# Bucketed attention before two feed-forward layers: q and k brought feature first, one-hot rows replaced by sign-bit rows, scores copied to SBUF by VectorE

## The chip, the cores and the metric

The kernel runs on one core of one Trainium2 chip. The metric is the device time of one execution in microseconds. The kernel before takes 830.13 us (median of three runs, 829.33 to 830.82).

## What is computed

For each of 2 x 8 heads of 768 rows and 64 features, a six-bit bucket is formed of every q row and every k row (the signs of six projections). Row i may attend to column j only if the buckets are equal. The result goes through two feed-forward layers of 1536 tokens, 512 to 2048 to 512.

```python
q_bits = (einsum('bhsd,dk->bhsk', q, proj) > 0)       # k_bits likewise
mask = q_bucket[:, :, :, None] == k_bucket[:, :, None, :]
scores = where(mask, scale * q @ k.T, -1e9)
attn = exp(scores - max(scores)); attn /= (attn.sum(-1) + 1e-9)
x = (attn @ v) heads side by side                     # (1536, 512)
h = x @ w_in;  g = where(h > 0, h, exp(min(h, 0)) - 1);  x = g @ w_out
h = x @ w_in2; g = s * relu(h) ** 2 + b;                 out = g @ w_out2
```

## The kernel before

Every fp32 product is made of fp32r parts: a value is split into `hi` (rounded to fp32r) and `lo` (the rest), and two or three products of parts are summed. Five engine programs are written by hand and meet at counting semaphores; the order on each engine is the order of the text.

**Units and pairs.** The attention part runs over 8 pairs of heads (`PAIRS`). A pair is 12 units (`UNITS`), six blocks of 128 query rows for each of its two heads; `k` is the unit in the pair, `u` the unit in all. In unit `k` TensorE does: the scores of unit `u + 2` (`AHEAD`), four matmuls of 384 columns (`scores`, L449); the transposes of the probabilities of unit `u`, six fp32 blocks of 128x128 in two groups of three (`transpose_probs`, L461); and then, by `third = k % 3`, either the turn of a finished value product (`turn`, L485; `third` 0) or half of the value product of the three units before (`times_v`, L470; six matmuls of 384 columns; `third` 1 and 2). A unit with the turn is called a turn unit here, the others value units.

**Buffers in PSUM.** `s_ps` has two buffers of two banks, `pt_ps` two of one bank, `pv_ps` and `prep_ps` one bank each: eight in all. Scores of `u` wait for the exponential of `u - 2` (L452).

**Per unit on the other engines.** VectorE takes the minimum of each row of the (negated) scores out of PSUM (`row_minimum`, L752), ScalarE reads the scores from PSUM again and writes the exponentials to `probs` (`exp`, L647, with the row sum as accumulator output). The transposed halves leave PSUM in two steps each: ScalarE copies `pt_hi` (L627), VectorE subtracts `pt_lo` (L759), so two pairs of evictions of 384 columns a unit.

**Preparation of the next head.** A table `PLAN` spreads eight cycles over three places of each unit: q and k are transposed through `prep_ps` (QA, QB, KA, KB: three fp32r transposes each, L429), projected (ZA, ZB: eight matmuls, L434), their signs stored as `bits` (L744), and two small bf16 products (EA, EB, L439) count the equal bits for every bucket; ScalarE makes one-hot rows of q (L640) and VectorE mismatch rows of k times 2^60 (L747), so that the score product itself adds 2^60 where the buckets differ. Three DMAs inside SBUF copy rows (`copy_hi`, L273). GpSimd (POOL) splits q, k and v and one block of feed-forward weights a pair. The x transposes (L446) bring a pair's result into `xt_hi` (ScalarE) and `xt_lo` (VectorE, L793), in units 3 and 9.

**End of a group.** After each three units VectorE inverts the row sums (`invert`, L765 and L767) and, behind the turn, multiplies them in (`normalise`, L776).

```python
        elif cycle <= ZB:
            for j, x in enumerate((qt1, qt1, kt2, kt2)):
                last = mm(dst, planes[:, n, j, :], x[par][:, cols], ...)
...
    ts(kt2[par][DH:P, cols], bank[0:BUCKETS, 0:HALF], equal_at, BIG, ALU.not_equal, ALU.mult)
...
    ts(row_inv[:, c], row_sum[:, c], EPS, None, ALU.add)
```

**The feed-forward layers** take 2304 matmuls of 512 columns (`hidden` L492, `output` L507). Four hidden blocks (12 matmuls each) of the first chunk are worked in at the end of the attention part, in units of the drain after the last pair (`FILL`, and one more behind the last x transposes). ScalarE and VectorE turn each hidden block into `g_hi` and `g_lo` (Relu, Exp, g, L877, L879), for which `output` waits.

Of the kernel before, what the change touches and what calls it, by code (L numbers as in the profile page):

```python
# [64 lines left out]

C_ID, C_II, C_CODE, C_THR, C_END = 0, P, P + DH, 2 * P + DH, 2 * P + DH + 1


def constants():

    c = np.zeros((P, C_END), np.float32)
    c[:, C_ID:C_ID + P] = np.eye(P)  # L90
    c[:, C_II:C_II + DH] = np.tile(np.eye(DH), (2, 1))
    bit = (np.arange(BUCKETS)[None, :] >> np.arange(BITS)[:, None]) & 1
    for start in (0, BIT_ROWS):
        c[start + BITS:start + 2 * BITS, C_CODE:C_CODE + BUCKETS] = 4 * bit - 2
        c[start:start + BITS, C_CODE + BUCKETS:C_CODE + 2 * BUCKETS] = 4 * bit - 2
    equal = BITS + (2 * bit - 1).sum(0)
    c[0:BUCKETS, C_THR] = equal
    c[BUCKETS:, C_THR] = 1 - equal
    return c

# [8 lines left out]
def build(nc, q, k, v, proj, consts, w1_in, w1_out, w2_in, w2_out, s2, b2, out):  # L109
    ctx = ExitStack()  # L110
    with ctx:
# [11 lines left out]
        ident_r = sb("ident_r", [P, P], F32R)  # L123
        code = sb("code", [P, P], BF16)
# [8 lines left out]
        equal_at = cst[0:BUCKETS, C_THR:C_THR + 1]  # L133
        onehot_bias = cst[BUCKETS:P, C_THR:C_THR + 1]
# [779 lines left out]
```

## Time and profile before

| | |
|---|---|
| median of 3 runs | 830.13 us (829.33 to 830.82) |
| span of the profiled execution, first to last instruction | 824.9 us |
| PE / DVE / ACT / POOL busy | 809.9 / 445.3 / 364.7 / 181.0 us |
| granted TensorE clock, mean | 1.000 of full speed |
| attention part | from the start to about 290 us |
| feed-forward layers | from about 290 us to the end |

The profile shows one execution. Its only time of its own is the span; what lies around it is not in the page, and the runs' median is 5.2 us above it. Busy shares are averages over two parts with different needs: in the attention part VectorE and ScalarE are busy for most of the time, in the layers for a third and a quarter of it.

### The profile page before, as it was taken

The page shows a single profiled execution, that of the slowest core. Times are in us where ns is not written, and L with a number is a line of the kernel's source. Part 1 is how long each engine was busy: PE and PEld are TensorE (multiplying, and loading weights), DVE is VectorE, ACT ScalarE, POOL GpSimd, SP SyncE. Part 2 cuts the span into 40 slices and gives each one's busy share as a digit, 9 for nine tenths or more (in the row PEclk, how much of TensorE's full clock was granted, in tenths as well). Part 3 has the DMA queues.
Part 4 walks back from the last instruction along what each step waited for, and adds up shares of the span by engine and source line. Part 5 has one row for each costly group of instructions (what it writes and reads, how often), then busy time and mean ns, then how long its engine had stood idle before and what let it go on. Part 6 is the DMA issues. An engine that isn't in the chain of part 4 may idle for free.

```text
span 824.9 us, 12868 instructions
## 1 busy us (share of the span) xinstructions
PE 809.9 (98%) x4252; PEld 697.6 (85%) x4252; DVE 445.3 (54%) x780; ACT 364.7 (44%) x735; POOL 181.0 (22%) x160
## 2 busy tenths in 40 slices
PE   7999999999999999999999999999999999999998
PEld 6799999999999977888888888887888888888886
DVE  6888888888888839533333343335223432243323
ACT  4888888888888831123221222213221222222221
POOL 3243332334322209400000036663000000000000
PEclk9999999999999999999999999999999999999999
DMA  3423243232323013200000012330000100010001
GB/s 97 120 59 94 76 103 91 57 92 74 87 68 88 1 52 125 80 1 0 1 1 1 0 33 94 102 102 26 1 1 0 51 0 0 0 51 0 0 0 51
DMA packets 34359, 38.70 MB, mean 47 GB/s; under 512 B 3168, under 2 KB 25824, under 8 KB 34336
## 3 DMA queue, kind: packets, MB, share of 16 engines
q1 hardware_dynamic: 33744, 38.22, 16.0%
q8 instruction: 15, 0.25, 0.1%
q10 hardware_dynamic: 592, 0.17, 0.1%
q14 instruction: 8, 0.07, 0.0%
HBM read 26.38 MB, written 3.15 MB: 36 GB/s over the span
## 4 chain that ended last, share of the span: by engine, by line
PE 94%; DVE 3%; DMA 1%; ACT 1%; issue 0%; SPq 0%; ACTq 0%; DVEq 0%
PE acc L521 31%; PE h_ps L503 31%; PE pt_ps L466 8%; PE s_ps L457 4%; PE pv_ps L479 4%; PE pv_ps L480 4%; PE s_ps L458 4%; PE prep_ps L434 2%; PE pv_ps L489 2%; PE prep_ps L429 2%; PE prep_ps L439 1%; DVE g_lo L879 1%; PE prep_ps L446 1%; DVE pt_lo L759 1%; DMA qt<-qt 0%
## 5 line engine op out<-in xcount | busy, mean ns | idle before, releaser
L721 ACT ACTIVATE r_sb<-h_ps 128x512 f32<-128x512 f32 x96 | 57.4, 598 | 359.4 <-PE h_ps L503 359.4
L873 DVE TENSOR_SCALAR g_sb<-e_sb,sb_scale 128x512 f32<-128x512 f32 x48 | 26.2, 546 | 158.1 <-ACT e_sb L724 158.1
L759 DVE TENSOR_TENSOR pt_lo<-pt_ps,pt_hi 128x384 fp32r<-128x384 f32 x192 | 103.4, 552 | 13.2 <-ACT pt_hi L627 11.3
L871 DVE SCALAR_TENSOR_TENSOR g_sb<-e_sb,h_ps 128x512 f32<-128x512 f32 x48 | 32.9, 686 | 132.2 <-ACT e_sb L724 132.2
L627 ACT ACTIVATE pt_hi<-pt_ps 128x384 fp32r<-128x384 f32 x192 | 93.4, 494 | 24.5 <-PE pt_ps L466 23.7
L752 DVE TENSOR_REDUCE row_min<-s_ps 128x1 f32<-128x768 f32 x96 | 91.4, 953 | 21.0 <-PE s_ps L458 20.5
L466 PE MATMUL pt_ps<-cst,probs 128*128 128x128 f32 x576 | 95.8, 277 | 1.5 <-DVE pt_lo L759 1.5
L647 ACT ACTIVATE probs<-s_ps,row_min 128x768 f32<-128x768 f32 x96 | 86.7, 904 | 0.9
L879 DVE TENSOR_TENSOR g_lo<-g_sb,g_hi 128x512 fp32r<-128x512 f32 x96 | 80.5, 838 | 3.3
L466 PEld LDWEIGHTS pt_ps<-cst,probs 128*128 128x128 f32 x576 | 68.6, 140 | 12.4 <-issue 6.0
L503 PE MATMUL h_ps<-xt_hi,wa_hi 128*128 (+1 forms) x192 | 75.1, 391 | 0.4 <-DVEq L856 0.4
L503 PE MATMUL h_ps<-xt_hi,wa_lo 128*128 (+1 forms) x192 | 74.8, 389 | 0.0
L503 PE MATMUL h_ps<-xt_lo,wa_hi 128*128 (+1 forms) x192 | 74.7, 389 | 0.0
L503 PE MATMUL h_ps<-xt_hi,wb_hi 128*128 (+1 forms) x192 | 74.7, 389 | 0.0
L503 PE MATMUL h_ps<-xt_lo,wb_hi 128*128 (+1 forms) x192 | 74.7, 389 | 0.0
L503 PE MATMUL h_ps<-xt_hi,wb_lo 128*128 (+1 forms) x192 | 74.7, 389 | 0.0
L479 PE MATMUL pv_ps<-pt_hi,v_nat 128*128 128x384 f32 x192 | 70.4, 366 | 0.6 <-DVE w_raw L776 0.6
L457 PE MATMUL s_ps<-kt,qt 128*128 128x384 f32 x192 | 68.4, 356 | 2.5 <-ACT qt L640 1.3
L724 ACT ACTIVATE e_sb<-r_sb 128x512 f32<-128x512 f32 x96 | 60.7, 632 | 11.0 <-ACT r_sb L721 0.8
L480 PE MATMUL pv_ps<-pt_lo,v_nat 128*128 128x384 f32 x192 | 64.8, 338 | 0.0
L458 PE MATMUL s_ps<-kt,qt 128*128 128x384 f32 x192 | 64.5, 336 | 0.0
L361 POOL CAST wa_hi<-w_raw 128x1024 f32 (+1 forms) x16 | 17.6, 1103 | 157.1 <-PE acc L521 157.1
(118 smaller groups left out, 1613.2 us busy)
## 6 DMA issues: line engine op xcount, KB each, us to landing
w_raw<-w_in_dram SPq DMA_DIRECT2D x32, 256.0 KB, 2.8
w_raw<-w_out_dram SPq DMA_DIRECT2D x32, 256.0 KB, 2.9
kt<-kt SPq DMA_DIRECT2D x30, 192.0 KB, 2.9
raw_q<-q_dram SPq DMA_DIRECT2D x16, 192.0 KB, 2.4
raw_k<-k_dram SPq DMA_DIRECT2D x16, 192.0 KB, 2.5
raw_v<-v_dram SPq DMA_DIRECT2D x16, 192.0 KB, 2.4
out_dram<-o_sb SPq DMA_DIRECT2D x12, 256.0 KB, 2.1
qt<-qt SPq DMA_DIRECT2D x15, 192.0 KB, 3.7
```

What stands on the lines that cost most here:

```text
L457: mm(s_ps[buf][:, n, 0:HALF], q1, kt1[par][:, cols], start=True, stop=False)
L458: last = mm(s_ps[buf][:, n, 0:HALF], q2, kt2[par][:, cols], start=False, stop=True)
L466: last = nc.tensor.transpose(pt_ps[n][:, r * P:(r + 1) * P], probs[k % 2][:, (n * HT + r) * P:(n * HT + r + 1) * P], ident)
L479: mm(pv_ps[:, 0:HALF], v_nat[par][:, kt, :], pt_hi[buf][:, kt, :], start=kt == 0, stop=False)
L480: last = mm(pv_ps[:, 0:HALF], v_nat[par][:, kt, :], pt_lo[buf][:, kt, :], start=False, stop=kt == TILES - 1)
L503: last = mm(bank[:], w[a][:, kt * P:(kt + 1) * P], x[b], start=n == 0, stop=n == 3 * KT - 1)
L521: last = mm(acc[n][:], lhs, rhs, start=f == 0 and j == 0, stop=f == FT - 1 and j == 2)
L627: return nc.scalar.activation(dst, src, ACT.Copy, scale=scale)
L647: nc.scalar.activation(probs[k % 2][:].rearrange("p (n c) -> p n c", n=2), s_ps[k % 2][:, :, 0:HALF], ACT.Exp, bias=row_min[:, k:k + 1], s ...
L752: nc.vector.tensor_reduce(row_min[:, k:k + 1], s_ps[k % 2][:, :, 0:HALF], AX.XY, ALU.min).then_inc(min_done, 1)
L759: tt(pt_lo[(k // HT) % 2][where], pt_ps[n][:, 0:HALF].rearrange("p (t c) -> p t c", t=HT), pt_hi[(k // HT) % 2][where].bitcast(F32), ALU.s ...
L879: tt(lo[:], g[:], hi[:].bitcast(F32), ALU.subtract).then_inc(g_ready, 1)
```

## The change

- **Host.** q and k arrive transposed and one under the other (`qk`, 64 rows of k, 64 rows of q, 768 columns), v and the planes of the projection laid out. One load a head instead of two.
- **TensorE** loses the q and k transposes, two of the eight projection matmuls a head (`project`: planes_hi and planes_lo by kt1, planes_hi by kt2) and the one-hot products. `project` stands at the end of units 1 and 7, the x transposes at the end of units 4 and 5.
- **Masking.** Instead of one-hot rows, twelve rows of sign bits times 2^31 lie in `qt2` and `kt2`; their product adds 2^62 for every bit that differs. VectorE writes them in four instructions of 12x384 (`write_bits`, units 2, 3, 8 and 9).
- **Scores.** `s_ps` has one buffer of two banks. VectorE copies the scores to `probs` (three buffers) under a ceiling of 2^60 and gives the row minimum as accumulator output of the same instruction (`keep_scores`); ScalarE takes the exponential in place, from SBUF. Scores of `u` wait for `keep_scores` of `u - 1`.
- **Evictions.** `pt_ps` has two buffers of two banks; a unit has one copy `pt_hi` and one subtraction `pt_lo` of 768 columns.
- **Moves.** `normalise` goes from VectorE (one instruction) to ScalarE (three of 64 columns); x is kept by ScalarE as fp32 (`keep_x`) and split by GpSimd (`split_x`); GpSimd scales q, splits q and k together. The inverse's first step becomes a scalar_tensor_tensor with a second tensor of zeros.
- **SP** copies q's high part twice, q's low part and k's high part once a head.
- **Ends.** Head 0 is split by ScalarE and VectorE in place; the last pair takes hidden blocks 0 and 1 in the place of scores, and blocks 2 and 3 around the last turns; none stands behind the last x transposes.

```diff
-        s_ps = [pb(f"s_ps{n}", [P, 2, 512], att_ps) for n in range(2)]
-        pt_ps = [pb(f"pt_ps{n}", [P, 512], att_ps) for n in range(2)]
+        s_ps = pb("s_ps", [P, 2, 512], att_ps)
+        pt_ps = [pb(f"pt_ps{n}", [P, 1024], att_ps) for n in range(2)]
...
 # GpSimd
+                nc.gpsimd.tensor_scalar(raw[low, :], raw[low, :], -SCALE, 1.0, ALU.mult, ALU.mult).then_inc(q_scaled, 1)
+                wait(pool, scores_done, TILES * (head - 1))
+                nc.gpsimd.tensor_copy(kt1[par][:], raw[:]).then_inc(qk_hi, 1)
+                nc.gpsimd.tensor_tensor(kt2[par][:], raw[:], kt1[par][:].bitcast(F32), ALU.subtract).then_inc(qk_split, 1)
...
 # TensorE
-                wait(pe, exp_done, u - 1)
+                wait(pe, scores_kept, u)
...
+                    if (k + AHEAD) % TILES == 0:
+                        pe.wait_ge(q_copied, 48 * head)
+                        pe.wait_ge(k_copied, 16 * head)
+                        pe.wait_ge(bits_done, 4 * head + 3)
+                    if (k + AHEAD) % TILES == HT:
+                        pe.wait_ge(bits_done, 4 * head + 4)
...
 # ScalarE
+                if third == 1 and not (first and k < 2 * HT):
+                    normalise(i, k // HT - 2)
+                if k < UNITS - 1 or more:
+                    exp(u + 1, (k + 1) % UNITS)
+                if third == 0 and not (first and k < 2 * HT):
+                    keep_pv(i, k // HT - 2)
+                split_hi(u, k)
+                if k in X_UNIT and not first:
+                    keep_x(i - 1, X_UNIT[k])
...
 # VectorE
+                ts(dst[DH:DH + 2 * BITS, n * HALF:(n + 1) * HALF], prep_ps[rows, 0:HALF], cst[rows, C_THR:C_THR + 1],
+                   BIT_SIZE, ALU.is_gt, ALU.mult).then_inc(bits_done, 1)
...
+                ts(probs[k % SRING][:].rearrange("p (n c) -> p n c", n=2), s_ps[:, :, 0:HALF], CEILING, HUGE, ALU.min,
+                   ALU.min, accum_out=row_min[:, k:k + 1]).then_inc(scores_kept, 1)
...
-                ts(row_inv[:, c], row_sum[:, c], EPS, None, ALU.add).then_inc(inv_step, 1)
+                nc.vector.scalar_tensor_tensor(row_inv[:, c], row_sum[:, c], EPS, zeros, ALU.add, ALU.add).then_inc(sum_done, 1)
...
+                    keep_scores(u + AHEAD, (k + AHEAD) % UNITS)
+                if blocks:
+                    write_bits(2 * i + off, off % 2, blocks[0])
+                split_lo(u, k)
+                if blocks:
+                    write_bits(2 * i + off, off % 2, blocks[1])
+                if third == 2:
+                    invert(i, k // HT)
```

How the order moves, first on VectorE. Before, units 1 and 2 of a pair (here the last), from the row minimum of unit 1 to the inverse of unit 2:

```order
L752 TENSOR_REDUCE row_min<-s_ps 128x1
L759 TENSOR_TENSOR pt_lo<-pt_ps,pt_hi 128x3x128
L747 TENSOR_SCALAR kt_1<-prep_ps,cst 64x384
L759 TENSOR_TENSOR pt_lo<-pt_ps,pt_hi 128x3x128
L752 TENSOR_REDUCE row_min<-s_ps 128x1
L759 TENSOR_TENSOR pt_lo<-pt_ps,pt_hi 128x3x128
L747 TENSOR_SCALAR kt_1<-prep_ps,cst 64x384
L759 TENSOR_TENSOR pt_lo<-pt_ps,pt_hi 128x3x128
L765 TENSOR_SCALAR row_inv<-row_sum 128x3
L767 RECIPROCAL row_inv<-row_inv 128x3
```

After, units 2 and 3 of the last pair, all that VectorE does in them:

```order
L721 TENSOR_SCALAR probs,row_min<-s_ps 128x768
L714 TENSOR_SCALAR kt_1<-prep_ps,cst 12x384
L728 TENSOR_TENSOR pt_lo<-pt_ps,pt_hi 128x6x128
L714 TENSOR_SCALAR kt_1<-prep_ps,cst 12x384
L734 SCALAR_TENSOR_TENSOR row_inv<-row_sum,cst 128x3
L736 RECIPROCAL row_inv<-row_inv 128x3
L721 TENSOR_SCALAR probs,row_min<-s_ps 128x768
L714 TENSOR_SCALAR qt_1<-prep_ps,cst 12x384
L728 TENSOR_TENSOR pt_lo<-pt_ps,pt_hi 128x6x128
L714 TENSOR_SCALAR qt_1<-prep_ps,cst 12x384
```

The four instructions that make a head's mask rows now stand in two neighbouring units instead of three, and the third of them, for which TensorE waits in unit 4, stands behind two copies of scores, a subtraction and the inverse.

Then TensorE: unit 0 of the last pair before, with the projection of the next head between transposes and turn,

```order
L466 MATMUL pt_ps<-cst,probs 128x128 x3
L434 MATMUL prep_ps<-qt_1,planes 128x384 x2
L434 MATMUL prep_ps<-kt_1,planes 128x384 x2
L466 MATMUL pt_ps<-cst,probs 128x128 x3
L489 MATMUL pv_ps<-cst,pv_sb 128x64 x3
L434 MATMUL prep_ps<-qt_1,planes 128x384 x2
L434 MATMUL prep_ps<-kt_1,planes 128x384 x2
```

and after, the end of unit 1, where the projection now stands (the rows before it are the transposes and the value matmuls of that unit):

```order
L448 MATMUL pt_ps<-cst,probs 128x128 x6
L461 MATMUL pv_ps<-pt_hi,v_nat 128x384
...
L416 MATMUL prep_ps<-kt_1,planes_hi 128x384
L417 MATMUL prep_ps<-kt_1,planes_lo 128x384
L416 MATMUL prep_ps<-kt_1,planes_hi 128x384
L417 MATMUL prep_ps<-kt_1,planes_lo 128x384
L422 MATMUL prep_ps<-kt_1,planes_hi 128x384 x2
```

The projection moved from unit 0 to the end of unit 1 and reads kt_1 alone, in which k and q now lie together.

## Rows read from the trace of the kernel before

**Rows 1.** The page: the span
```profile
span 824.9 us, 12868 instructions
```

**Rows 2.** Windows, 150 to 190 us: us busy (instructions), clock, DMA
```profile
core 0: us, PE busy (x) PEld busy (x) DVE busy (x) ACT busy (x) POOL busy (x), PEclk, DMA share, GB/s
150.00:190.00 40.00, 40.00 (x283) 37.54 (x282) 33.75 (x64) 33.65 (x77) 16.88 (x18) 1.00 0.32 87
```

**Rows 3.** Timeline, PE: start us, length us, engine, line, operation, out<-in, count
```profile
141.08 0.34 PE L457 MATMUL s_ps<-kt,qt 128*128 128x384 f32 x1
146.74 0.34 PE L457 MATMUL s_ps<-kt,qt 128*128 128x384 f32 x1
147.76 0.49 PE L446 MATMUL prep_ps<-cst,w_raw 128*128 128x128 f32 x3
148.09 0.49 PE L466 MATMUL pt_ps<-cst,probs 128*128 128x128 f32 x3
149.00 0.42 PE L457 MATMUL s_ps<-kt,qt 128*128 128x384 f32 x1
176.11 0.34 PE L457 MATMUL s_ps<-kt,qt 128*128 128x384 f32 x1
...
280.83 0.34 PE L457 MATMUL s_ps<-kt,qt 128*128 128x384 f32 x1
281.01 0.34 PE L458 MATMUL s_ps<-kt,qt 128*128 128x384 f32 x1
283.25 0.34 PE L457 MATMUL s_ps<-kt,qt 128*128 128x384 f32 x1
```

**Rows 4.** Timeline, DVE at 146 to 148 us, PE and DVE at 162 us
```profile
146.26 0.61 DVE L747 TENSOR_SCALAR kt<-prep_ps,cst 64x384 fp32r<-64x384 f32 x1
146.90 0.56 DVE L759 TENSOR_TENSOR pt_lo<-pt_ps,pt_hi 128x384 fp32r<-128x384 f32 x1
147.38 0.18 DVE L765 TENSOR_SCALAR row_inv<-row_sum 128x3 f32<-128x3 f32 x1
147.69 0.96 DVE L752 TENSOR_REDUCE row_min<-s_ps 128x1 f32<-128x768 f32 x1
...
161.82 0.34 PE L458 MATMUL s_ps<-kt,qt 128*128 128x384 f32 x1
162.19 0.96 DVE L752 TENSOR_REDUCE row_min<-s_ps 128x1 f32<-128x768 f32 x1 [0.16 <-PE s_ps L458]
```

**Rows 5.** Timeline, POOL, 147 to 149 us
```profile
147.04 0.50 POOL L352 CAST v_nat<-raw_v 128x384 fp32r<-128x384 f32 x1 [13.21 <-PE pv_ps L480]
147.62 1.00 POOL L354 TENSOR_TENSOR v_nat<-raw_v,v_nat 128x384 fp32r<-128x384 f32 x1
148.57 0.50 POOL L335 CAST q_nat<-raw_q 128x384 fp32r<-128x384 f32 x1
```

**Rows 6.** Timeline, POOL and DVE, then tile g_lo (ns, min/median/max)
```profile
312.76 2.40 POOL L363 TENSOR_TENSOR wb_lo<-w_raw,wb_hi 128x1024 f32 x1 [0.17 <-POOL wb_hi L361]
312.91 2.80 DVE L879 TENSOR_TENSOR g_lo<-g_sb,g_hi 128x512 fp32r<-128x512 f32 x1
L879 DVE TENSOR_TENSOR g_lo<-g_sb,g_hi x96: 691/693/2803, 306.8 to 816.0; 128x512 fp32r<-128x512 f32 x96
```

**Rows 7.** Groups of instructions: total busy us, mean ns of one, idle before
```profile
L647 ACT ACTIVATION_READ_ACCUMULATOR probs<-s_ps,row_min 128x1 f32 x96 | 19.5, 203 | 0.0
```

**Rows 8.** Timeline of the start: first cast of q, first and third unit's score matmuls
```profile
4.37 0.36 DVE L820 CAST q_nat<-raw_q 128x384 fp32r<-128x384 f32 x1 [0.21 <-DMA raw_k<-k_dram]
12.67 0.41 PE L457 MATMUL s_ps<-kt,qt 128*128 128x384 f32 x1 [1.27 <-ACT qt L640]
16.50 0.44 PE L457 MATMUL s_ps<-kt,qt 128*128 128x384 f32 x1 [1.21 <-ACT probs L647]
```

**Rows 9.** Timeline, PE: the first output matmul of the feed-forward layers
```profile
307.53 0.50 PE L521 MATMUL acc<-g_hi,wa_hi 128*128 128x512 f32 x1 [0.95 <-DVE g_lo L879]
```

**Rows 10.** The page's DMA issues: count, KB each, us to landing
```profile
kt<-kt SPq DMA_DIRECT2D x30, 192.0 KB, 2.9
```

More of the change, by code:

```diff
@@ L91, in constants, with laid_planes @@
     c[:, C_II:C_II + DH] = np.tile(np.eye(DH), (2, 1))
[L92 to L98, printed above, removed]
-    return c
+    for start in range(0, P, 2 * BIT_ROWS):
+        c[start + BITS:start + 2 * BITS, C_THR] = -TINY
+        c[start + BIT_ROWS:start + BIT_ROWS + BITS, C_THR] = -TINY
+    return c
+def laid_planes(proj):
+    c = np.zeros((P, 2, 2, P), np.float32)
+    for n in range(2):
+        q, k = n * 2 * BIT_ROWS, n * 2 * BIT_ROWS + BIT_ROWS
+        for first, sign in ((0, -1), (BITS, 1)):
+            for rows, at in ((slice(DH, P), q + first), (slice(0, DH), k + first)):
+                c[rows, 0, n, at:at + BITS] = proj
+                c[rows, 1, n, at:at + BITS] = sign
+    return c.reshape(P, 4 * P)
 def wait(eng, sem, value):
@@ L300, in _ @@
                 pair(i)
[L301 to L304 removed]
+            pair(PAIRS - 2, after=False)
+            pair(PAIRS - 1, nxt=False, after=False)
             sp.wait_ge(xt_pe, 2 * PAIRS)
@@ L577, in _ @@
+                if k in Z_UNIT and (more or Z_UNIT[k] < 2):
+                    if k > TILES and not first:
+                        pe.wait_ge(x_kept, 2 * i)
+                    project(2 * i + Z_UNIT[k], Z_UNIT[k] % 2)
             pe.wait_ge(zeros_ready, 1)
@@ new lines, in keep_pv, with normalise @@
+            def keep_pv(i, g):
+                act.wait_ge(pv_done, GROUPS * i + g + 1)
+                copy(pv_sb[:], pv_ps[:, 0:HALF]).then_inc(pv_copied, 1)
+            def normalise(i, g):
+                par, G, first = (g % GROUPS) // 2, GROUPS * i + g, (g % GROUPS) * HT
+                act.wait_ge(inv_done, G + 1)
+                act.wait_ge(pv_turned, G + 1)
+                if g in (0, 1):
+                    wait(act, xt_pe, 2 * i - 1 + g)
+                for r in range(HT):
+                    last = copy(x_nat[:, (g % 2) * HT + r, par * DH:(par + 1) * DH], pv_ps[:, r * DH:(r + 1) * DH],
+                                row_inv[:, first + r:first + r + 1])
+                last.then_inc(x_done, 1)
@@ new lines, in _ @@
+            nc.scalar.activation(row_sum[:, 0:1], qk_scale[:], ACT.Exp)
+            act.wait_ge(k0_in, 16)
+            act.wait_ge(q0_in, 16)
+            for n in range(2):
+                cols = slice(n * HALF, (n + 1) * HALF)
+                copy(kt1[0][:, cols], raw[:, cols], qk_scale[:]).then_inc(hi0_done, 1)
+            act.wait_ge(hi0_done, 2)
+            copy(qt1[0][top, :], kt1[0][low, :].bitcast(F32)).then_inc(q0_copied, 1)
+            copy(qt2[0][top, :], kt1[0][low, :].bitcast(F32)).then_inc(q0_copied, 1)
@@ L709, in _ @@
                 unit(PAIRS - 1, k, more=False)
-            for k in range(X_UNIT[1] + 1):
-                unit(PAIRS, k, main=False)
+            keep_pv(PAIRS, -2)
+            normalise(PAIRS, -2)
+            keep_pv(PAIRS, -1)
+            keep_x(PAIRS - 1, 0)
+            normalise(PAIRS, -1)
+            keep_x(PAIRS - 1, 1)
             for layer in range(2):
@@ L846, in _ @@
+            for block in range(4):
+                write_bits(0, 0, block)
             for k in range(AHEAD):
-                row_minimum(k, k)
+                keep_scores(k, k)
             for k in range(UNITS):
```

604 lines of the change are left out of this document (248 added, 356 removed).

## The prediction, made before the changed kernel ran

> **What bounds the kernel now.** I read the windows first, then TensorE's timeline, then VectorE's. In 40 us of the attention part TensorE is busy for all 40.00 us at a granted clock of 1.00 (the 2.4 GHz level), VectorE for 33.75, ScalarE for 33.65, GpSimd for 16.88 [rows 2]. The chain of waits, followed back from the end, runs almost wholly over PE. So TensorE bounds the kernel, and VectorE and ScalarE stand only 16% behind it. The period is read where the same score matmul comes back one pair of heads later: 141.08 to 176.11, 35.03 us for 12 units [rows 3]. The two feed-forward layers (2304 matmuls, from about 290 us on) are untouched but for their first waits; I take them as equal. The sum is made against the profiled span, 824.9 us [rows 1]; the median of the runs, 830.13, is 5.2 above it, and I add 5.2 at the end.
>
> **TensorE's work after the change.** A unit without extras that ends in value matmuls takes 283.25 - 280.83 = 2.42 us. A unit that ends in the turn takes 2.26 (146.74 to 149.00) with three x transposes in it, which cost 0.33 (147.76 to 148.09), so 1.93 without. The first score matmul behind the fp32 turn lasts 0.42 instead of 0.34, 0.09 more with its start; score matmuls follow each other every 0.175 us [rows 3]. Per pair: 4 turn units 7.72, 8 value units 19.36, 4 transitions 0.36, two projections of 6 matmuls 2.10, two groups of x transposes, each now followed by a transition, 0.84. Together 30.4 us, against 35.03: the q and k transposes, two of eight projection matmuls a head, the one-hot matmuls and their transitions give back **4.65 us a pair**. Were TensorE still the bound this would be some 35 us in all.
>
> **The new wait: bits before scores.** The order rows show it. Scores of the next head begin in unit 4 (and 10) and want three of the four bit blocks. The third stands on VectorE behind, from the start of unit 2: keep_scores, bits, split_lo, bits, the inverse, keep_scores, bits. Step by step from the first score matmul of unit 2:
> - the four score matmuls end at 3 x 0.175 + 0.34 = 0.87, VectorE starts 0.03 later (161.82 + 0.34, then 162.19) [rows 4]: 0.90;
> - keep_scores, 128x768 out of PSUM, is not in the trace. The nearest is the row minimum of the same elements, 0.96 [rows 4]; nothing shows it cheaper or dearer than by a tenth either way; I take 0.95: 1.85. It now also gives an accumulator. A separate read may follow: between nothing and ScalarE's 0.203 [rows 7]; I take 0.09: 1.94;
> - bits: the old kt instruction, also with a pointer operand, 0.61, starting only when its predecessor has ended and letting its successor start 0.03 after its own end (146.26, 146.90) [rows 4]: 1.97 to 2.58;
> - split_lo of 768 elements in place of two of 384: 0.95, as the row minimum: 3.56. ScalarE is not late: transposes end at about 1.5, one eviction of 768 (some 0.8) at 2.4;
> - bits to 4.20; inverse and reciprocal, from 147.38 to the next start at 147.69 [rows 4], 0.31: 4.54; keep_scores with its read to 5.58; bits to 6.22; TensorE sees it at 6.27.
>
> TensorE has by then only 2.42 + 1.93 = 4.35 us of work. It waits **1.9 us a head**, 3.8 a pair. Nothing hides it: the score bank is single now, so TensorE cannot run ahead.
>
> **Smaller new waits.** With one score bank, scores of u+1 wait for keep_scores of u. Behind the inverse of units 11 and 5 VectorE is late by the same reckoning by 0.4 and 0.3: 0.7 a pair. In unit 6 the turn waits for pv_sb, since ScalarE has keep_x, the exponential (now out of SBUF) and keep_pv in a row: about 0.6. Sum of waits 5.1, so a pair takes 30.4 + 5.1 = 35.5 us against 35.03: +0.45, times 7 pairs **+3.2**.
>
> **Costed at nothing.** ScalarE loses the q, k and one-hot evictions and gains three 64-column normalisations a group; by the sum it is busy some 80% and stays hidden. POOL's split of raw (768 columns, so twice 0.50 and twice 1.00 from [rows 5], and a scaling of about 1 us) is over some 6 us after its v split starts, while its projection stands four to five units later. SP has four copies a head instead of three and one load instead of two; the last copy (kt1, 2.9 us median to landing [rows 10]) starts at the end of unit 1 and is wanted 6.2 us later. If that cover went, the scores of units 4 and 10 would wait for it instead of the bits.
>
> **Ends.** Start: the first scores come at 12.67 and the third at 16.50 now [rows 8]. The loads of q were ready at 4.37 and k's with them [rows 8]. After: the low part is split behind the planes at about 6.8, its projection ends at 7.2, POOL's copy of q's low part lets the bits start at 7.9, three bits end at 9.85. With the same 3.8 to 4 us of ramp the third scores come at 13.9: **-2.6** (0 to -4). The old kernel did half of head 1's preparation before unit 0, and the second half of its last pair was free of preparation, which was worth more there than it is now: **+1.5**. Tail: from the last scores, 283.25, to the first output matmul, 307.53, are 24.3 us now, the last 0.95 of it a wait for g_lo [rows 3, 9]. After: four hidden blocks of 12 matmuls at 0.175 x 512/384, 2.8 each, the rest of three units 5.4, turns 1.2, the last 12 value matmuls 2.2, x groups 0.8, in all 20.8 of work, and waits of 0.4, 0.4 and 0.8 in the pv and x steps and 3.7 before the first output, since no hidden block is left to stand over the chain keep_x, Relu, Exp, g, g_hi, g_lo: 26.1, **+1.8**.
>
> Sum: 3.2 + 1.5 + 1.8 - 2.6 = +3.9: span 828.8, with 5.2 **834 us**.
>
> **The lock on the inverse (rival 1, slower still).** The inverse was a tensor_scalar with one SBUF operand; at 147.38 it ran while GpSimd was busy (147.04 to 147.54) and took its usual time [rows 4, 5]. Now it is a scalar_tensor_tensor with two SBUF operands. The nearest instruction with two is g_lo: 0.69 us as a rule, but 2.80 when it met GpSimd's subtraction of 2.40, ending 0.55 after that one [rows 6]. In the new order GpSimd's scaling would start, by 147.04 (0.30 into the unit behind the last value matmul) and the two v steps of 1.53 [rows 5], 2.42 + 0.30 + 1.53 = 4.25 us after unit 2's start; the inverse is due at 4.23. If it comes second it waits for about 1 us (0.5 to 1, 64 partitions of 768), and so does the third bit: 15 heads x 0.95 = +14: **848 us**. Between "never" and "at both heads" a few hundredths decide, so I hold it nearly as likely as the forecast. The Trainium skill (SBUF — State Buffer, section "SBUF: two separate sides") says the port pair of VectorE and GpSimd is an exclusive lock, also against a two-SBUF-input VectorE instruction; the trace agrees (2.80 against 0.69).
>
> The Trainium skill (VectorE: DVE Perf Modes, "Two Vector instructions with no wait between them") counts an instruction with an accumulator output as two, which speaks against keep_scores; no VectorE row shows one. By ScalarE's full 0.203 instead of 0.09 the sum would be 837, and with no read 831.
>
> **Rival 2, the other sign.** The VectorE chain is shorter than the rows of the old instructions say: no accumulator read (2 x 0.09) and its six joints overlap by 0.1 each, as split_lo and the inverse do (146.90, 0.56 long, and 147.38 [rows 4]). That is -0.8 a head, -12: **822 us**. It decides from about 0.35 us a head on. Against it: 146.26 to 146.90 shows no overlap around such an instruction.
> **Rival 3.** The waits hardly come, TensorE stays full: 834 less 5.1 x 7.5 = **796 us**. The window rows speak for it (VectorE has less busy time in sum), the order rows against.
> **Rival 4.** POOL or SP deliver late, or the longer gaps of the start drop the clock: **842 or more**. The slack of 6 us and a clock of 1.00 throughout speak against.
>
> **Numbers.** Forecast (834, its own range 828 to 839) 0.42, rival 1 (839 to 849) 0.31, rival 2 (815 to 828) 0.16, rival 3 0.07, rival 4 0.04. The range takes the forecast, rival 1 and most of rival 2: 819 to 849; outside stay rival 3, a part of 2 and of 4. A measurement tells 0.2% (828.5 to 831.8) from no change. Faster 0.24, same 0.10 (the low end of the forecast), slower 0.66.
>
> **What would show it.** In the windows of 150 to 190 us PE should be busy for about 34 of 40, its idle time ending at the first score matmul of units 4 and 10 on the bits (a TENSOR_SCALAR of 12x384), 1.9 us each; a pair should last 35.5 us; keep_scores 0.95, perhaps with a read row; the third scores near 14 us; the wait for the first g_lo 3.7 us. SCALAR_TENSOR_TENSOR row_inv of 0.17 us says no lock, of 1 us lock and waits of 2.8. The forecast is wrong if PE waits less than 1.5 us a head there, if the instruction 12x384 or keep_scores is far from 0.61 and 0.95, or if PE waits for DMA or POOL.

## The result, and the profile after

The changed kernel takes **846.37 us** in the median (846.25 to 847.2, 4 runs) against 830.06 us (829.33 to 830.82, 4 runs): a ratio of 1.0203, 95% interval 1.0189 to 1.0218. It is slower by 16.3 us; the forecast was slower by 3.9. One execution of e3_order ran in a slow state, at a mean clock of 0.84, took 901.7 us and is left out of its figures.

The page of the changed kernel: the span, busy time of each engine, and the granted clock in 40 slices of 21 us each.

```profile
span 845.4 us, 11759 instructions
PE 794.2 (94%) x3996; PEld 690.2 (82%) x3996; DVE 432.0 (51%) x734; ACT 337.2 (40%) x643; POOL 216.2 (26%) x182
PEclk6899999999999998999999999999999999999999
```

TensorE has 16 us less to do than before and the span is 20 us longer. The clock row, which was full throughout before, begins with 6 and 8, and a 9 in this row stands for anything from 0.9 up, so it can hide a short loss: windows of 5 us find five of them in slices marked 9. The windows say how much. The first row answers to [rows 2]; the other two are of the start:

```profile
150.00:190.00 40.00, 35.65 (x230) 34.15 (x230) 31.02 (x55) 28.25 (x62) 18.92 (x18) 0.96 0.32 82
0.00:10.00 10.00, 5.57 (x18) 4.61 (x18) 3.59 (x8) 5.02 (x7) 3.51 (x11) 0.90 0.42 116
10.00:22.00 12.00, 8.78 (x29) 7.39 (x30) 6.08 (x11) 3.78 (x7) 6.30 (x7) 0.51 0.44 114
```

PE is busy for 35.65 of 40 us instead of 40.00, and at a clock of 0.96 instead of 1.00; at the start it runs for 12 us at half of its speed (the 1.2 GHz level), and once more around the wait of 4.34 us for the bits of the second head (0.50 in the window of 30 to 35 us).

The waits of PE from 36 to 300 us (what it waited for: us in total, times, longest):

```profile
PE s_ps L440 <- DVE qt L714: 24.6, 14, 1.9
PE pv_ps L471 <- ACT pv_sb L595: 3.6, 7, 0.5
PE s_ps L440 <- DVE probs L721: 2.2, 7, 0.4
```

Fourteen waits for the bits (`qt`, L714), 1.75 us each; seven for pv_sb, 0.5 each; seven for keep_scores (`probs`), 0.3 each. These are the three waits that the prediction named, and there is no fourth. The chain behind the first of them, VectorE's timeline in units 2 and 3 and the score matmul that waited (start, length, engine, line):

```profile
154.55 0.96 DVE L721 TENSOR_SCALAR_CACHE_REDUCE probs<-s_ps 128x768 f32<-128x768 f32 x1 [0.76 <-PE s_ps L441]
155.44 0.08 DVE L721 DVE_READ_ACCUMULATOR probs<-s_ps 128x1 f32 x1
155.55 0.61 DVE L714 TENSOR_SCALAR kt<-prep_ps,cst 12x384 fp32r<-12x384 f32 x1
156.20 0.96 DVE L728 TENSOR_TENSOR pt_lo<-pt_ps,pt_hi 128x768 fp32r<-128x768 f32 x1
157.19 0.62 DVE L714 TENSOR_SCALAR kt<-prep_ps,cst 12x384 fp32r<-12x384 f32 x1
157.84 0.16 DVE L734 SCALAR_TENSOR_TENSOR row_inv<-row_sum,cst 128x3 f32<-128x3 f32 x1
158.04 0.18 DVE L736 RECIPROCAL row_inv<-row_inv 128x3 f32<-128x3 f32 x1
158.25 0.96 DVE L721 TENSOR_SCALAR_CACHE_REDUCE probs<-s_ps 128x768 f32<-128x768 f32 x1
...
159.25 0.61 DVE L714 TENSOR_SCALAR qt<-prep_ps,cst 12x384 fp32r<-12x384 f32 x1
...
159.99 0.44 PE L440 MATMUL s_ps<-kt,qt 128*128 128x384 f32 x1 [1.74 <-DVE qt L714]
```

VectorE works without a break from 154.55 to 159.86, and the matmul starts 0.13 us later. The same wait in another pair is followed by something else:

```profile
85.52 0.44 PE L440 MATMUL s_ps<-kt,qt 128*128 128x384 f32 x1 [1.74 <-DVE qt L714]
86.33 1.25 PE L448 MATMUL pt_ps<-cst,probs 128*128 128x128 f32 x6
87.69 0.52 PE L462 MATMUL pv_ps<-pt_lo,v_nat 128*128 128x384 f32 x1
88.01 0.52 PE L461 MATMUL pv_ps<-pt_hi,v_nat 128*128 128x384 f32 x1
...
90.89 0.43 PE L461 MATMUL pv_ps<-pt_hi,v_nat 128*128 128x384 f32 x1
91.15 0.34 PE L462 MATMUL pv_ps<-pt_lo,v_nat 128*128 128x384 f32 x1
```

From 86.5 to about 90 us the matmuls follow each other every 0.32 us instead of 0.175: the chip has gone to its lower clock. Of the 14 gaps five were followed by such a stretch, and each cost 1.4 to 1.6 us (a pair with one against the pairs without).

Marks of the program, each the start of a matmul in PE's timeline, for the executions that the text compares (us):

| | first scores | second pair's | last pair's | last scores | first output | end |
|---|---|---|---|---|---|---|
| before | 12.67 | 43.92 | 254.10 | 283.25 | 307.53 | 824.9 |
| before, again (e11) | 13.96 | 46.82 | 257.10 | 286.24 | 310.49 | 828.0 |
| changed | 11.01 | 50.08 | 270.19 | 302.34 | 328.77 | 845.4 |
| e6_warm_ends | 11.09 | 45.97 | 259.92 | 290.62 | 317.04 | 832.2 |
| e9_spread_behind | 11.35 | 44.04 | 237.16 | 265.89 | 292.07 | 809.5 |
| e10_spread_ends | 11.05 | 41.10 | 234.25 | 262.99 | 287.55 | 802.5 |

Changed against before, stage by stage: first pair with the start +6.2 us, the six pairs behind it +9.9 (220.11 against 210.18), the last pair +3.0, from the last scores to the first output +2.1, the layers -0.7: +20.5 in the spans. The six pairs lasted 35.44, 37.14, 37.33, 37.30, 35.74 and 37.16 us.

### The profile page after: what moved, and what is told of

The parts are those of the page before. It is cut to its first block, busy times and chain, and to the rows that moved or that the text cites. A ratio compares the mean times of both kernels' runs of the same rounds, so it can differ in the third digit from the quotient of the medians.

```text
span 845.4 us, 11759 instructions
## 1 busy us (share of the span) xinstructions
PE 794.2 (94%) x3996; PEld 690.2 (82%) x3996; DVE 432.0 (51%) x734; ACT 337.2 (40%) x643; POOL 216.2 (26%) x182
## 4 chain that ended last, share of the span: by engine, by line
PE 85%; DVE 7%; issue 5%; ACT 2%; DMA 0%; DVEq 0%; POOL 0%; SPq 0%; ACTq 0%
PE acc L505 31%; PE h_ps L487 31%; PE pt_ps L448 5%; PE s_ps L440 4%; PE pv_ps L461 3%; PE pv_ps L462 3%; PE s_ps L441 3%; DVE kt L714 2%; DVE pt_lo L728 1%; DVE probs L721 1%; DVE qt L714 1%; PE pv_ps L471 1%; ACT probs L600 1%; PE prep_ps L429 1%; PE prep_ps L422 1%
## 5 line engine op out<-in xcount | busy, mean ns | idle before, releaser
L728 DVE TENSOR_TENSOR pt_lo<-pt_ps,pt_hi 128x768 fp32r<-128x768 f32 x96 | 92.0, 958 | 39.2 <-ACT pt_hi L595 37.6
L595 ACT ACTIVATE pt_hi<-pt_ps 128x768 fp32r<-128x768 f32 x96 | 77.9, 812 | 75.6 <-PE pt_ps L448 75.3
L721 DVE TENSOR_SCALAR_CACHE_REDUCE probs<-s_ps 128x768 f32<-128x768 f32 x96 | 91.9, 958 | 29.2 <-PE s_ps L441 26.0
L440 PE MATMUL s_ps<-kt,qt 128*128 128x384 f32 x192 | 72.3, 376 | 36.2 <-DVE qt L714 31.3
L600 ACT ACTIVATE probs<-probs,row_min 128x768 f32<-128x768 f32 x96 | 89.7, 934 | 11.3 <-DVE probs L721 11.1
L448 PE MATMUL pt_ps<-cst,probs 128*128 128x128 f32 x576 | 82.8, 282 | 0.0
L810 DVE TENSOR_TENSOR g_lo<-g_sb,g_hi 128x512 fp32r<-128x512 f32 x96 | 74.9, 780 | 3.3
L448 PEld LDWEIGHTS pt_ps<-cst,probs 128*128 128x128 f32 x576 | 72.2, 146 | 3.9
L461 PE MATMUL pv_ps<-pt_hi,v_nat 128*128 128x384 f32 x192 | 74.0, 386 | 0.0
L440 PEld LDWEIGHTS s_ps<-kt,qt 128*128 128x128 f32 x192 | 38.2, 199 | 41.8 <-DVE probs L721 28.0
L441 PE MATMUL s_ps<-kt,qt 128*128 128x384 f32 x192 | 67.1, 349 | 0.0
```

The costliest lines, as they stand in the source:

```text
L440: mm(s_ps[:, n, 0:HALF], q1, kt1[par][:, cols], start=True, stop=False)
L441: last = mm(s_ps[:, n, 0:HALF], q2, kt2[par][:, cols], start=False, stop=True)
L448: last = nc.tensor.transpose(pt_ps[k % 2][:, r * P:(r + 1) * P], probs[k % SRING][:, r * P:(r + 1) * P], ident)
L461: mm(pv_ps[:, 0:HALF], v_nat[par][:, kt, :], pt_hi[buf][:, kt, :], start=kt == 0, stop=False)
L595: return nc.scalar.activation(dst, src, ACT.Copy, scale=scale)
L600: nc.scalar.activation(probs[k % SRING][:], probs[k % SRING][:], ACT.Exp, bias=row_min[:, k:k + 1], scale=-1.0, accum_out=row_sum[:, k:k + ...
```

## The experiments

Theory A: the waits are VectorE's chain, as forecast, and the rest of the time is the clock that the gaps cost. Rivals: the clock falls for another reason (B); something else stands right behind the bits (C); GpSimd's port holds VectorE up according to the form of the instruction (L). All kernels are the changed one with the edit named; the kernel before had 829 to 830 us in each comparison.

### Filling the gap, first attempt: e1_fill, and the start too: e2_warm

```diff
                     if (k + AHEAD) % TILES == 0:
+                        pe.wait_ge(scores_kept, u + AHEAD)
+                        for _ in range(FILL):
+                            mm(s_ps[:, 0, 0:2 * P], planes_hi[:, 0:P], planes_hi[:, 0:2 * P], start=True, stop=True)
                         pe.wait_ge(q_copied, 48 * head)
```

e2_warm adds matmuls of zeros (function `warm`) in the start's gaps.

> Only the gap is filled: before TensorE waits for the bits (units 4 and 10) it does 14 matmuls of 256 columns (about 1.6 us) whose result is overwritten by the scores. Theory A (the time beyond the forecast is the clock: each wait of 1.7 us for the bits can be followed by a stretch at the 1.2 GHz level, 1.6 us lost each time): every pair from the second on lasts 35.4 to 35.8 us, the granted clock is 1.00 from 40 to 320 us, and the time falls by 6 to 8 us to 838 to 841. Theory B (the clock falls have another cause, such as the total load or the DMAs): the lower stretches stay and the time is 846 to 849.

> As e1_fill, and the gaps of the start are filled too: 17 instead of 12 matmuls of zeros at the very start, 13 behind the first projection, 5 behind each of the first two units of scores, 34 instead of 14 fillers at the first wait for bits. Theory A: the start too runs at the 2.4 GHz level, the first pair shrinks from 39.1 us by 2 to 4, the time is 834 to 838. Theory B (the start is bound by loads, VectorE and GpSimd, not by TensorE's clock): the clock is 1.00 there, but the time is within 1 us of e1_fill. If fillers delay the real matmuls: above e1_fill.

Measured: e1_fill 853.73 us (ratio to before 1.0287, 1.0259 to 1.0314), e2_warm 852.46 (1.0268, 1.0239 to 1.0297). Neither theory had foreseen slower than the changed kernel. The trace of e1_fill shows why:

```profile
163.74 1.93 PE L520 MATMUL s_ps<-planes_hi 128*128 128x256 f32 x14 [1.02 <-DVE probs L725]
165.51 0.34 PE L441 MATMUL s_ps<-kt,qt 128*128 128x384 f32 x1
```

The filler writes s_ps, so it had to wait for keep_scores, 1.02 us; the gap was over when it had hardly begun, and it then stood in the way of the scores for 1 us, 15 times. The steady pairs last 37.5 us each, in e2_warm too, at a clock of 1.00. So the clock could be kept up, but by a filler that cost more than the clock. The attempt says nothing about the price; e5 repeats it in the right place.

### Filling the gap where it is: e5_fill_gap and e6_warm_ends

```diff
+                if (k + AHEAD + 1) % TILES == 0 and (k < TILES or more):
+                    pe.wait_ge(pt_lo_done, u)
+                    for _ in range(FILL):
+                        mm(pt_ps[(k + 1) % 2][:, SEQ:1024], planes_hi[:, 0:P], planes_hi[:, 0:2 * P], start=True, stop=True)
```

> The filler of e1_fill stood behind keep_scores and ran on past the end of the gap; here 12 matmuls of 256 columns (1.5 us) stand right behind the turn of units 3 and 9, in a part of pt_ps that nobody reads, and end before the bits are written. Nothing else is changed. Theory A (clock): the bits come when they did, no stretch of the pairs runs at 1.2 GHz any more, each pair from the second lasts 35.4 to 35.8 us (four of them lasted 37.1 to 37.3), the time falls by 6 to 8 us to 838 to 841. Theory B (the lower clock comes from something else than the gap): falls stay, 846 or more.

> As e5_fill_gap, with the gaps of both ends filled too: the start as in e2_warm, 28 fillers instead of 12 at the first wait for bits, 24 before the first output matmul. Theory A: the clock is 1.00 throughout; what this kernel is below the changed one is the whole price of the clock: 4 to 5 us at the start (unit 4 of the first pair came at 19.7 instead of 22.9 us in e2_warm), 1.8 at the first output, 6 to 8 in between: 832 to 836. Theory B: the start is bound by VectorE, GpSimd and loads: within 1.5 us of e5_fill_gap.

Measured: e5_fill_gap **839.18 us** (838.95 to 839.87), e6_warm_ends **834.02** (833.81 to 834.29; ratio to before 1.0053, 1.0035 to 1.0071). Windows of e6_warm_ends, the start and the rest of the attention part:

```profile
0.00:36.00 36.00, 30.19 (x177) 27.36 (x177) 24.98 (x43) 19.63 (x35) 16.00 (x21) 1.00 0.46 123
36.00:320.00 284.00, 272.24 (x1825) 258.15 (x1826) 217.19 (x387) 198.03 (x413) 116.70 (x115) 1.00 0.31 79
```

and of the changed kernel over the second stretch:

```profile
36.00:320.00 284.00, 253.41 (x1628) 241.60 (x1627) 215.78 (x387) 194.47 (x407) 112.98 (x110) 0.97 0.30 76
```

The useful work is the same, and the bits come at the same point of a pair; in e5_fill_gap the steady pairs last 35.72, 35.75, 35.74, 35.71 and 35.75 us. What goes is the stretches at the lower clock: 7.2 us with the gaps of the pairs filled and 12.35 us with both ends. Theory A holds, and B falls. At the start the row of the clock is not enough to judge by. In e5_fill_gap, where the start is not filled, it shows 1.00 from 10 to 20 us, and yet the score matmuls there last 0.52 us, as they do in the changed kernel, whose row shows the lower clock:

```profile
10.00:20.00 10.00, 6.44 (x19) 5.14 (x20) 4.69 (x9) 2.36 (x6) 6.28 (x7) 1.00 0.52 130
11.81 0.52 PE L442 MATMUL s_ps<-kt,qt 128*128 128x384 f32 x1
```

So the recorded clock can lack a slow stretch. In e6_warm_ends the matmuls themselves are at full speed there (0.34 us). The table of marks shows where the 13.2 us between the spans of the changed kernel and e6 lie: 4.1 up to the second pair, 6.2 in the six pairs, 1.5 in the last pair, 1.5 behind the first output. That last one is a wait, too:

```profile
328.77 0.80 PE L505 MATMUL acc<-g_hi,wa_hi 128*128 128x512 f32 x1 [3.72 <-DVE g_lo L810]
329.79 0.63 PE L505 MATMUL acc<-g_hi,wa_lo 128*128 128x512 f32 x1
...
332.57 0.40 PE L505 MATMUL acc<-g_hi,wa_hi 128*128 128x512 f32 x1
```

The matmuls behind it follow each other every 0.43 us until 332.3 instead of every 0.23.

### What the bits cost in all: e4_no_bits

```diff
+                if not first:
+                    dve.nop().then_inc(bits_done, 1)
+                    return
                 ts(dst[DH:DH + 2 * BITS,
```

> VectorE writes the sign-bit rows of head 0 alone; for the other 15 heads it counts the semaphore only (the masks of those heads are left out). It prices all of the bits on VectorE. Theory A: the waits of 1.74 us a head go (26 us) and with them the clock falls (8): 805 to 815 us, a pair lasts 31 to 32 us, TensorE is the bound again. Theory C (scores wait for the DMA copies or POOL anyway): over 830.

Measured: 811.31 us (810.94 and 811.68), a pair 32.27 us, the clock 1.00 from the second pair on, no wait for bits. Without them PE waits for pv_sb (0.5 a pair) and keep_scores (0.3 a pair) alone. So the bits' chain and what it does to the clock are worth 35 us; POOL, the third copy and ScalarE were early enough, and C falls.

### VectorE's order: e3_order, and with the old inverse: e8_order_ts

```diff
+                if blocks and blocks[0] == 0:
+                    write_bits(2 * i + off, off % 2, 0)
                 if k < UNITS - AHEAD or more:
                     keep_scores(u + AHEAD, (k + AHEAD) % UNITS)
...
+                if third == 0 and not (first and k == 0):
+                    invert(i, k // HT - 1)
                 split_lo(u, k)
...
-                if third == 2:
-                    invert(i, k // HT)
```

> VectorE's order alone: the first bits of unit 2 stand ahead of keep_scores (in the time in which the scores are being made), and each inverse stands one unit later, behind keep_scores (and behind the third bits). Theory A (the wait is the sum of the VectorE chain): the wait of units 4 and 10 falls from 1.74 to 0.7 us, the waits for keep_scores behind the inverse of units 5 and 11 go (0.35 each): 1.4 us a head, 21 in all, less what pv_sb keeps: a pair lasts 33 to 33.5 us and the time is 822 to 830, lower still where the shorter wait leaves the clock at 1.00. Theory C (another releaser stands right behind the bits: the third DMA copy, POOL's split, pv_sb): the wait changes its name and the time falls by less than 8 us (838 or more). The moved inverse now falls into GpSimd's split of q and k, where it may take 1.6 us, as it did once at 27 us; that would be off TensorE's path.

> As e3_order, and the inverse is again the tensor_scalar with one SBUF operand of the kernel before. In e3_order the form with two SBUF operands took 0.57 us in the median and up to 2.17 where it met GpSimd's split of q and k. Theory L (two SBUF operands wait for GpSimd, one does not): it takes 0.18 us everywhere, the extra wait for keep_scores one unit later (3.23 against 2.55 us between scores) goes, a pair falls from 35.2 to 33.9 to 34.4 us, the time from 833.7 to 823 to 828. Rival (the moved inverse is late for another reason): over 832.

Measured: e3_order 833.72 us (833.03 to 834.07), e8_order_ts 832.42 (831.58 to 833.79). The first is 12.7 us below the changed kernel, short of the 16 to 24 expected. Its pair lasts 35.2 us, the wait for bits is 1.19 us (expected 0.7), and the unit behind each of these waits got slower, 3.23 us between its scores against 2.55. VectorE's timeline of e3_order says why:

```profile
201.26 0.96 DVE L728 TENSOR_TENSOR pt_lo<-pt_ps,pt_hi 128x768 fp32r<-128x768 f32 x1 [0.49 <-ACT pt_hi L595]
202.25 0.62 DVE L714 TENSOR_SCALAR kt<-prep_ps,cst 12x384 fp32r<-12x384 f32 x1
...
203.91 0.61 DVE L714 TENSOR_SCALAR qt<-prep_ps,cst 12x384 fp32r<-12x384 f32 x1
204.27 0.83 POOL L320 CAST kt<-raw 128x768 fp32r<-128x768 f32 x1
204.54 0.57 DVE L734 SCALAR_TENSOR_TENSOR row_inv<-row_sum,cst 128x3 f32<-128x3 f32 x1
```

The second bits stand behind a subtraction that now waits 0.49 us for ScalarE's copy; the time won ahead of keep_scores is lost there. And the moved inverse meets GpSimd's cast: it takes 0.57 us and ends with it (205.11 and 205.10). More than half of the gain was the clock, 7.6 of 13.4 us in the spans: the gaps of 1.2 us were never followed by a slow stretch, in 14 cases here and 14 in e8, where five of 14 gaps of 1.74 were.

e8 puts the old form back and expected that to free the inverse. Two meetings in its trace, the instruction and what GpSimd does at that time:

```profile
141.10 0.82 DVE L734 TENSOR_SCALAR row_inv<-row_sum 128x3 f32<-128x3 f32 x1
151.29 0.58 DVE L734 TENSOR_SCALAR row_inv<-row_sum 128x3 f32<-128x3 f32 x1
158.90 0.16 DVE L734 TENSOR_SCALAR row_inv<-row_sum 128x3 f32<-128x3 f32 x1
...
140.91 0.99 POOL L331 TENSOR_TENSOR xt_lo<-x_raw,xt_hi 128x384 f32 x1 [0.17 <-POOL xt_hi L329]
151.02 0.82 POOL L320 CAST kt<-raw 128x768 fp32r<-128x768 f32 x1
```

The first two end 0.02 and 0.03 us behind GpSimd's instruction (141.92 and 141.90, 151.87 and 151.84); the third meets none and takes 0.16. The form with one SBUF operand waits as the other does: a median of 0.572 us in e8, 0.567 in e3. Theory L falls, and the pair is 35.2 us with either. So the rival to L had the time right (over 832), and the cause of the late inverse is GpSimd all the same.

### Room on VectorE: e7_spread, e9_spread_behind

```diff
-Z_UNIT = {1: 1, TILES + 1: 2}
+Z_UNIT = {0: 1, TILES: 2}
```

In e7 the bits stand in unit 1 ahead of keep_scores and behind it, and ahead of it in units 2 and 3 (and the same six units later). In e9 VectorE's units 1 to 3 read

```
 unit 1:  write_bits 0, keep_scores, write_bits 1, split_lo
 unit 2:  keep_scores, invert, write_bits 2, split_lo
 unit 3:  keep_scores, split_lo, write_bits 3
```

and `invert` waits for the exponential itself (`dve.wait_ge(exp_done, HT * (G + 1))`), since it stands ahead of the subtraction that implied it.

> The projection stands one unit earlier (end of units 0 and 6) and the four instructions for the bits in units 1 (two: ahead of keep_scores and behind it), 2 (one, ahead) and 3 (one, ahead); the inverse stays. Theory A (the wait is VectorE's chain between projection and scores): scores of units 4 and 10 wait 0 to 0.3 us for bits; a pair lasts 32.3 (as with no bits) to 33 us and the time is 811 to 819. Theory C (VectorE has no room for the bits anywhere, since it was busy 34.8 of 40 us with them in e3_order): the wait moves to keep_scores, a pair lasts 34 us or more, the time is over 824.

> As e7_spread, but no bits ahead of keep_scores where VectorE is already late: the third instruction stands behind keep_scores in unit 2, the fourth behind the subtraction in unit 3; and the inverse of each group stands ahead of the subtraction, before GpSimd's split of v begins. Theory A (VectorE's chain is the wait): unit 2 waits no longer (0.4), unit 3 waits 0.6 to 0.9 instead of 1.2, the inverse takes 0.16 us everywhere: a pair falls from 34.8 to 33.0 to 33.8 us, the time from 829.6 to 814 to 823, faster than both kernels. Rival (VectorE's load over units 1 to 3 is what counts, whatever its order): a pair stays at 34.5 or more, the time at 827 or more.

Measured: e7_spread 829.63 us (ratio 0.9999, 0.9988 to 1.0009). That is what its theory C gave (over 824, the wait moves to keep_scores, a pair of 34 us or more: it lasts 34.8), but C's reason, that VectorE has no room for the bits anywhere, falls with e9_spread_behind: it takes **811.33** (0.9788, 0.9772 to 0.9804), below the 814 to 823 that its theory A gave. PE's waits from 36 us to the last scores of e9:

```profile
PE s_ps L441 <- DVE probs L722: 3.8, 14, 0.3
PE pv_ps L472 <- ACT pv_sb L596: 3.6, 7, 0.5
```

The waits for bits, 24.6 us in the changed kernel, are gone, and a pair lasts 32.2 us (32.27 in e4_no_bits), although VectorE now writes all bits (windows, 150 to 190 us: it is busy for 36.12 of 40 us, TensorE for 38.70). e7 differs from e9 in VectorE's order alone: the third and fourth bits, and the inverse of every group. In e7 the fourth bits stood ahead of a keep_scores that was late already (PE waited 1.07 us behind it), and the inverse met GpSimd's split of v:

```profile
199.10 1.02 POOL L342 TENSOR_TENSOR v_nat<-raw_v,v_nat 128x384 fp32r<-128x384 f32 x1
199.38 0.76 DVE L734 SCALAR_TENSOR_TENSOR row_inv<-row_sum,cst 128x3 f32<-128x3 f32 x1
200.17 0.17 DVE L736 RECIPROCAL row_inv<-row_inv 128x3 f32<-128x3 f32 x1
```

### Both ends: e10_spread_ends

```diff
-            hidden(0, 0, 3)
             times_v(PAIRS, -1, range(TILES))
...
             transpose_x(PAIRS, 1)
+            hidden(0, 0, 3)
```

with the start's fillers of e6 (`WARM = 17`, then `warm(13)` behind the first projection and `warm(5)` behind each of the first two scores).

> As e9_spread_behind, with the start filled as in e6_warm_ends (17, 13, 5 and 5 matmuls of zeros) and the fourth hidden block behind the last x transposes, over the chain that ends in the first g_lo. Theory A: 3 to 4 us less at the start (the clock), 1.5 to 3.5 at the end (a wait of 3.7 us is covered by 2.8 of work, of which 1.0 comes back as a wait for the normalised x, and the slow stretch behind it goes): 5 to 7 us below e9_spread_behind. Theory B (VectorE and GpSimd set the start, and the tail's chain): 0 to 3 us below it.

Measured: **804.34 us** (804.25 to 804.39; ratio to before 0.9702, 0.9687 to 0.9717), 7.0 below e9. By the table 2.9 come up to the last pair, 1.6 from the last scores to the first output (24.56 against 26.18 us; the wait for g_lo is 1.0 instead of 3.7), 2.5 behind it, where the slow stretch is gone. This is the fastest version of the study, 3.0% below the kernel before and 5.0% below the changed one.

### The kernel before, again: e11_before_again

> The kernel before once more, unchanged, for its clock: the execution profiled first had a granted clock of 1.000 and a span of 824.9 us, 5.2 below the median time; in all later runs time and span differ by 1.8 to 2.1 us. Theory A: the usual execution of the kernel before also loses clock, at the start or at the turn to the layers: a span of 826 to 829 us with a clock of 0.991 to 0.998 and one or two stretches at 1.2 GHz before 320 us. Rival: the clock is 1.00 everywhere and the 3 us come from elsewhere.

Measured: 830.21 us, span 828.0, clock 0.994. Windows of its start and of the rest of the attention part:

```profile
10.00:22.00 12.00, 9.24 (x43) 8.06 (x41) 5.02 (x7) 5.04 (x11) 5.73 (x8) 0.64 0.27 66
36.00:320.00 284.00, 280.40 (x1882) 258.93 (x1881) 232.44 (x433) 223.56 (x495) 91.12 (x98) 1.00 0.28 74
```

This execution of the kernel before, with a time near the median, loses clock as well, at the start alone: it is 2.9 us later at the second pair than the one profiled first, and 3.1 at the end. The two profiles part at 5.1 to 5.3 us, where GpSimd splits v and VectorE splits k. In the one profiled first VectorE's cast of k begins at 5.25, 0.04 us ahead of GpSimd's, and takes 0.35 us, the subtraction behind it 0.74. In e11 GpSimd is first:

```profile
5.10 0.61 POOL L352 CAST v_nat<-raw_v 128x384 fp32r<-128x384 f32 x1 [4.64 <-DMA raw_v<-v_dram]
5.26 0.66 DVE L820 CAST k_nat<-raw_k 128x384 fp32r<-128x384 f32 x1
5.96 1.24 DVE L822 TENSOR_TENSOR k_nat<-raw_k,k_nat 128x384 fp32r<-128x384 f32 x1
7.26 0.71 PE L429 MATMUL s_ps<-ident_r,k_nat 128*128 128x128 f32 x6 [1.08 <-DVE k_nat L822]
```

TensorE then waits 1.08 us for k, and the slow stretches follow. This is read from two executions, not tried.

Time and span differ by 1.8 to 2.3 us in all runs of which both are known. The 5.2 us that the prediction added for "what lies around" the span were some 2 us of that and 3 us of luck: the execution profiled had kept the full clock and a span near the shortest on record. That the clock is what the median execution lacks is shown for e11 alone. Most executions of the kernel before agree (826.7 to 828.6 us at a mean clock of 0.997 to 1.000, 830.5 to 831.1 at 0.991 and 0.992), but three at 0.999 and 1.000 took 829.7 to 830.1; they left no trace, and as the recorded clock can lack a stretch, it stays open whether they lost clock too.

## Why the prediction was wrong

It had the sign, the wait that decides and its place; the size was wrong by a factor of four, although the result lies in the range of 819 to 849. The step that failed is the price of the gaps in TensorE's clock, a term that the sum did not have; the start was mis-sized besides.

- **The length of a pair: right, by two errors that cancel.** The pairs without a slow stretch last 35.44 to 35.75 us (forecast 35.5). The three waits came where they were expected and a little shorter: for the bits 1.74 us a head (1.9), for pv_sb 0.5 a pair (0.6), for keep_scores 0.3 once a pair (0.7 in two), in all 4.2 us in the pair from 50.08 to 85.52 us, against 5.1. PE was therefore idle for 4.35 of 40 us where the forecast had some 6. TensorE's own work was longer: 31.26 us in that pair (31.16 in one of e9), against 30.4. Between the first score matmuls of units 2 and 4 it had 6.34 - 1.74 = 4.60 us of work, not 4.35. So the change gives TensorE back 3.8 us a pair and not 4.65.
- **The chain on VectorE: right.** The wait for the first g_lo is 3.72 (3.7). The bits take 0.61 as taken. From keep_scores to the start of the next instruction are 1.00 us (154.55 to 155.55), 0.07 less than the sum had with its read row; the two steps of the inverse take 0.41 instead of 0.31. The chain from the first score matmul of unit 2 to that of unit 4 (153.65 to 159.99) is 6.34 us long, forecast 6.27. The joints do not overlap, so rival 2 had nothing to live on. e3 to e9 agree with a chain: what was taken off it came back at TensorE, unless another wait stood in it.
- **The clock: the step that failed.** It stood in rival 4 (a chance of 0.04) as "the longer gaps of the start drop the clock", with "a clock of 1.00 throughout" against it. But that row was of an engine that was never idle in the pairs; the change itself made gaps of 1.74 us every 17 to 20 us, and no term priced what they do to the clock. What the runs show in its place: 12.35 us between the changed kernel and e6_warm_ends, 7.2 of them with the gaps of the pairs alone (e5_fill_gap). If the median execution of the kernel before pays the 3 us that e11 paid, 9 of the 16.3 us are the clock. The rest is 7.3 us, the difference of the spans of e6_warm_ends and of the kernel before at its full clock, where 3.9 stood: +2.05 up to the second pair, +3.8 in the six pairs, +1.55 in the last, +2.1 in the tail, -2.2 in the layers.
- **The reference execution.** The sum was made against a span with a full clock, 3 us shorter than that of an execution near the median, and then carried to the median. It hid part of the miss: forecast 828.8 as a span, e6_warm_ends 832.2 without any loss of clock, although both times read 834.
- **Start and first pair: mis-sized.** "Third scores at 13.9, -2.6": they came at 16.48, and at 15.20 in e6 with the clock kept. Then the first inverse of the changed kernel met GpSimd's subtraction, as rival 1 describes, and ended 0.02 us behind it:

```profile
26.87 1.80 POOL L322 TENSOR_TENSOR kt<-raw,kt 128x768 fp32r<-128x768 f32 x1
27.09 1.60 DVE L734 SCALAR_TENSOR_TENSOR row_inv<-row_sum,cst 128x3 f32<-128x3 f32 x1
```

Even with the full clock (e6) the second pair begins 2.05 us later than before, where the forecast had it earlier by about 2. The last pair is 1.55 us longer than before (30.70 against 29.15): "+1.5" for both ends covered this one alone. The tail, +1.8, was right (+2.1). The layers, taken as equal, are 2.2 us shorter in e6; 1.2 of that is a second wait for g_lo that the kernel before has at 311.75 us and e6 has not.
- **Rival 1, the lock: right number, wrong cause.** 848 us is near the result, but the inverse took 0.15 to 0.16 us in the steady pairs of the changed kernel. It fell into the seam between two of GpSimd's instructions: it ended at 158.00, the subtraction of v at 157.97, and the scaling began at 158.11, a miss of a tenth, as the working had left open. And its reason for the old form being safe was misread: at 147.38 [rows 4, 5] the instruction ended 0.02 us behind the cast, so it had no time to show a wait. e8 shows that form waiting for as long as the other. The Trainium skill (SBUF — State Buffer, "SBUF: two separate sides") names also VectorE instructions in a two-port mode as taking the lock; the 0.57 to 0.83 us of e8's tensor_scalar agree with a lock against it (whether it ran in such a mode, no row shows), and the prediction had taken the sentence for the two-operand case alone.
- **Rival 3** (TensorE stays full, 796) is what the idea comes near to with another order on VectorE: e9 and e10 reach 811 and 804. The 796 counted on 30.4 us of work a pair; there are 31.2.

What stays open: why five of the 14 gaps were followed by a slow stretch and nine were not; which of the orders changed between e7 and e9 gives how much, as the reasons were read from the trace and not tried piece by piece; and what the slower executions of the kernel before with a recorded clock near 1.00 lost.

## What to carry to other kernels

A wait on an engine that was full before has two prices, its length and the clock behind it; here the second was 7 us for the gaps of the pairs and 12 with both ends, three times the whole forecast, and dummy matmuls in the gaps bought it back. They must not write what TensorE still waits for: in the wrong place they cost 7 us (e1_fill). When steps move to an engine with room "on average", write out the two or three units around the consumer's deadline in order: nearly the same instructions gave 846, 830 or 811 us by their places. And compare the profiled execution's span and clock with several runs before its offset is carried anywhere.

## What the hardware showed unexpectedly

- A gap of 1.74 us in an otherwise busy TensorE was followed, in five of 14 cases, by some 3.5 us at 1.2 GHz (clock 0.66 in the window of 85 to 90 us); gaps of 1.2 us never were (28 of them in e3 and e8), nor gaps of 0.25 to 0.4 us (e5, e6).
- The recorded clock can lack a slow stretch: 1.00 from 10 to 20 us of e5_fill_gap, with score matmuls of 0.52 us there instead of 0.34.
- In two executions of the same kernel VectorE's cast began 0.04 us before GpSimd's or 0.16 behind it, and the spans differ by 3.1 us (the kernel before, and e11).
- VectorE's tensor_scalar on three columns of fp32, one SBUF operand, waits for a running GpSimd cast or subtraction and ends 0.02 to 0.03 us behind it (0.57 to 0.83 us instead of 0.16).
- A tensor_scalar with an accumulator output shows as two rows, 0.96 and 0.08 us, of which the second begins 0.07 us before the first ends; the next instruction starts 0.04 us behind the end of the first, so the accumulator cost nearly nothing.
